# A three-stage transformer kernel: the first and the last expert in half tiles by sequence

## What is computed

```python
def reference(**kwargs):
    attn_out = _attn_ref(**attn_kwargs)      # decayed linear attention, 8 heads of 64
    x = attn_out.transpose(0, 2, 1, 3).reshape(B, S, H * D)
    x = _moe_ref(x=x, **moe_kwargs)          # 8 experts, one for each token
    return _moe2_ref(x=x, **moe2_kwargs)     # 4 softmax attentions, the best 2 mixed

# _moe_ref, for each token s of sequence b:
            e = fresh_e if (s == 0 or local_gate[b, s] < 0.5) else prev_e
            h = np.maximum(x[b, s] @ w1[e], 0.0)
            out[b, s] = p[e] * (h @ w2[e])
```

## Time and profile before

| | us |
|---|---|
| median of 3 runs | 450.05 (449.87 to 450.38) |
| the profiled execution, its time | 451.0 |
| the same, its span from first to last instruction | 449.5 |
| PE busy in it | 409.4 (91%) |
| DVE, ACT, POOL busy | 255.6, 220.8, 78.3 |

### The profile page before, as it was taken

One profiled execution on the slowest core, in us unless ns is written; L12 is line 12 of the kernel. 1 busy time (PEld: TensorE's weight loads), 2 busy tenths in 40 slices (PEclk: granted clock), 3 DMA queues, 4 the chain that ended last, 5 costly groups with the idle time before them and its releaser, 6 DMA issues.

```text
span 449.5 us, 9492 instructions
## 1 busy us (share of the span) xinstructions
PE 409.4 (91%) x3224; PEld 365.5 (81%) x3225; DVE 255.6 (57%) x493; ACT 220.8 (49%) x460; POOL 78.3 (17%) x100
## 2 busy tenths in 40 slices
PE   6998896298999999999999999299899899989987
PEld 5887784297999999898989897299887789987875
DVE  1766777776464646464646465236777531677750
ACT  3644443254464645454545455134666553466643
POOL 1011112111010100000000000540178400025330
PEclk9999997579999999999999999789999999999999
DMA  8967693777877677767766850462200021220003
GB/s 263 364 184 244 210 399 162 244 248 237 280 240 263 232 260 240 253 234 271 233 234 233 267 201 23 135 170 71 71 1 2 1 95 49 70 70 0 0 0 140
DMA packets 32392, 77.47 MB, mean 172 GB/s; under 512 B 3824, under 2 KB 4080, under 8 KB 32368
## 3 DMA queue, kind: packets, MB, share of 16 engines
q1 hardware_dynamic: 25552, 57.94, 38.1%
q0 software_dynamic: 4224, 14.68, 9.5%
q10 hardware_dynamic: 2592, 4.53, 2.7%
HBM read 56.17 MB, written 17.83 MB: 165 GB/s over the span
## 4 chain that ended last, share of the span: by engine, by line
PE 75%; issue 11%; DMA 6%; DVE 3%; POOL 2%; ACT 1%; POOLq 1%; SPq 0%; ACTq 0%; DVEq 0%
PE bank L1220 7%; PE bank L1221 6%; PE bank L1222 6%; PE bank L1207 6%; PE bank L1206 6%; PE bank L1205 6%; PE bank L1324 5%; PE bank L1309 4%; PE bank L1291 3%; PE bank L1295 3%; PE bank L1266 2%; PE bank L1265 2%; PE bank L1267 2%; POOL tokens_by_expert L446 2%; DMA tokens_by_expert<-zero 2%
## 5 line engine op out<-in xcount | busy, mean ns | idle before, releaser
L1205 PE MATMUL bank<-xh,w1h 128*128 128x256 f32 x256 | 73.6, 288 | 0.9 <-DVE xl L886 0.9
L1206 PE MATMUL bank<-xl,w1h 128*128 128x256 f32 x256 | 73.5, 287 | 0.0
L1207 PE MATMUL bank<-xh,w1l 128*128 128x256 f32 x256 | 73.5, 287 | 0.0
L880 DVE TENSOR_TENSOR w2l<-raw,w2h 128x1024 fp32r<-128x1024 f32 x32 | 37.1, 1221 | 42.6 <-ACT w2h L560 42.6
L560 ACT ACTIVATE w2h<-raw 128x1024 fp32r<-128x1024 f32 x32 | 31.7, 1051 | 47.6 <-PE bank L1222 45.7
L1205 PEld LDWEIGHTS bank<-xh,w1h 128*128 128x128 f32 x256 | 50.3, 196 | 1.3 <-DVE xl L886 1.0
L1220 PE MATMUL bank<-w2h,hh 128*128 128x512 f32 x128 | 50.7, 396 | 0.0
L1206 PEld LDWEIGHTS bank<-xl,w1h 128*128 128x128 f32 x256 | 50.2, 196 | 0.3
L1207 PEld LDWEIGHTS bank<-xh,w1l 128*128 128x128 f32 x256 | 50.2, 196 | 0.0
L1222 PE MATMUL bank<-w2h,hl 128*128 128x512 f32 x128 | 49.9, 390 | 0.0
L1221 PE MATMUL bank<-w2l,hh 128*128 128x512 f32 x128 | 49.9, 389 | 0.0
(11 more groups left out here) (159 smaller groups left out, 859.8 us busy)
## 6 DMA issues: line engine op xcount, KB each, us to landing
raw<-in_w SPq DMA_DIRECT2D x64, 512.0 KB, 6.0
tokens_by_expert<-zero POOLq DMA_DIRECT2D x8, 512.0 KB, 6.2
xr<-tokens_by_expert POOLq DMA_DIRECT2D x8, 512.0 KB, 4.0
outputs_by_expert<-ysb ACTq DMA_DIRECT2D x16, 256.0 KB
kt_in<-in_kT SPq DMA_DIRECT2D x12, 256.0 KB
q_in<-in_qT SPq DMA_DIRECT2D x12, 256.0 KB
out<-osb SPq DMA_DIRECT2D x12, 256.0 KB, 2.0
v_in<-in_vR SPq DMA_DIRECT2D x11, 256.0 KB, 5.2
```

The lines of the kernel that those rows point to most:

```text
L880: dve.tensor_tensor(part(low), raw[:, q, :], part(high).bitcast(F32), ALU.subtract).then_inc(w_lo, 1)
L1205: pe.matmul(to, w1h[:, dc, at], xh[:, dc, :], start=(dc == 0), stop=False)
L1206: pe.matmul(to, w1h[:, dc, at], xl[:, dc, :], start=False, stop=False)
L1207: last = pe.matmul(to, w1l[:, dc, at], xh[:, dc, :], start=False, stop=(dc == DC - 1))
```

## The change

- Places: expert 7's tokens of sequence 0 and of sequence 1 go to two regions; expert 0's tokens of sequence 1 begin at row 128 at the earliest, so that its first 128 rows hold tokens of sequence 0 only. There are nine units (NU = 9) instead of eight experts: expert 0, experts 1 to 6, expert 7 for sequence 0, expert 7 for sequence 1. Units 0, 7 and 8 are taken in half tiles of 128 tokens, the others in tiles of 256 as before. The routing numbers have three links more in DVE's chain and tables of 99 entries instead of 48.
- The first half tile: SP loads it when sequence 0's six scatters have landed, and then expert 0's w1 into `raw` and w2 into `first_w2` (the place of `w2l`). PE turns it before the last block's output and multiplies it by the unsplit weights in full fp32, with the tokens as the stationary operand: 8 products of 512 columns for h (`first_h`) and 8 for y (`first_y`), spread between the last products of stage A and behind them. Since h now comes out with tokens on the partitions, ACT writes relu(h) to `hs` and PE turns it (`turn_hidden`, 4 transposes for each half of the hidden columns).
- A half tile of the loops (`half_loop`) is 24 split products of 512 columns for h, 8 transposes of `hs`, 8 of the next tile, and 24 products for y. The first 4 of the hidden transposes stand after 18 of the h products, the others after 3 of the y products.
- `ys` is two tensors, one for each sequence, in the order of tokens' places without gaps. Each tile is stored to both (unit 8 to sequence 1's alone), and a tile's surplus rows are overwritten by the next tile's store, so stores wait for the one before. The five zero fills of `ys` that SP issued in stage A go to POOL, behind its first tile load (`clear_outputs`).
- ACT's `tile_out` now stands at the end of an expert's turn, behind the next w1 pieces and ahead of the next w2 pieces; it waits for both parts of y and issues two stores of 512 KB.
- POOL gathers sequence 0's rows when unit 7 is stored, sequence 1's when unit 8 is.
- Sequence 0's six blocks are turned into six banks instead of two: PE turns four of them (`AHEAD`), then the others between the values' products.

```diff
@@ -191,11 +237,15 @@
...
+        first_w2, w2l = sb_twice("first_w2", "w2l", [P, FB, D])
...
+        first_x, xh = sb_twice("first_x", "xh", [P, DC, TILE])
...
+        first_hidden, hh = sb_twice("first_hidden", "hh", [P, FB, TILE])
@@ -378,33 +445,41 @@
...
+            for j in range(C):
+                sp.wait_ge(scattered[j], 16)
+            sp.dma_start(xr[:, 0, :], rows(xs, 0, P)).then_inc(first_tile_in, 16)
             for q in range(4):
                 load_w1(0, q)
...
-                sp.wait_ge(scattered[s], 16 * NB // XRING)
-            sp.dma_start(xr[:, :, :], rows(xs, 0, TILE).rearrange("(a p) n -> p a n", p=P)).then_inc(first_tile_in, 16)
+            for q in range(4):
+                src = rows(w2, q * 2 * P, 2 * P).rearrange("(a p) n -> p a n", p=P)
+                sp.dma_start(first_w2[:, 2 * q:2 * q + 2, :], src).then_inc(first_w2_in[q], 16)
+            for j in range(C, NB):
+                sp.wait_ge(scattered[j], 16)
+            sp.wait_ge(tileT_done, 2)
+            sp.dma_start(xr[:, 0, :], rows(xs, P, P)).then_inc(second_tile_in, 16)
+            sp.wait_ge(h_done, 4)
+            for q in range(4):
+                sp.wait_ge(w_lo, q + 1)
+                load_w1(1, q)
             sp.wait_ge(pads_ready, 1)
-            r = sp.value_load(pad_i[0:1, 0:1], min_val=0, max_val=E * REGION - TILE)
@@ -447,47 +524,65 @@
...
+                    if first:
+                        with pool.If(j == 0):
+                            clear_outputs()
...
+            def clear_outputs():
+                for k in range(4):
+                    pool.dma_start(rows(ys[0], S + k * 2 * CLEAR, 2 * CLEAR).rearrange("(p a) n -> p (a n)", p=CLEAR),
+                                   zero[0:CLEAR, :]).then_inc(ys_cleared, 16)
+                pool.dma_start(rows(ys[1], B * S, P), zero[:, 0:D]).then_inc(ys_cleared, 16)
...
+            pool.wait_ge(ey_stored, 32 * tb + 32)
+            pool.sem_inc(all_stored, 1)
+            pool.wait_ge(all_stored, 1)
             gather(0)
+            pool.wait_ge(ey_stored, 32 * tb + 16 * nt + 32)
+            pool.sem_inc(all_stored, 1)
+            pool.wait_ge(all_stored, 2)
@@ -543,95 +639,164 @@
...
+            def first_hi(q):
+                act.wait_ge(raw_in[q], 16)
+                act.activation(w1h[:, q, :], raw[:, q, :], ACT.Copy).then_inc(w_hi, 1)
+
+            half_hi(0, 2, first_x)
             kept(len(GROUPS) - 2)
+            first_hi(0)
             token_rows(NB - 1)
+            first_hi(1)
             kept(len(GROUPS) - 1)
...
+            first_hi(2)
...
+            def tile_out(before, row):
+                act.wait_ge(ey_stored, 32 * before)
+                act.wait_ge(ey_done, 2 * before)
                 for th in range(TH):
...
                     act.activation(ysb[:, th, :], bank[:, 6 + th, :], ACT.Copy).then_inc(ey_ready, 1)
...
+                act.wait_ge(ey_ready, 2 * before)
+                for y in ys:
+                    act.dma_start(rows(y, row, TILE).rearrange("(a p) n -> p a n", p=P), ysb[:, :, :]).then_inc(ey_stored, 16)
...
+            hidden_rows(0, 0)
+            first_hi(3)
+            hidden_hi(0, 0, first_hidden)
+            hidden_rows(0, 1)
+            hidden_hi(0, 1, first_hidden)
+            for q in range(4):
+                at = slice(2 * q, 2 * q + 2)
+                act.wait_ge(first_w2_in[q], 16)
+                act.activation(w2h[:, at, :], first_w2[:, at, :], ACT.Copy).then_inc(w_hi, 1)
+            act.wait_ge(ey_done, 2)
+            half_hi(1, 4, xh)
+            half_out(1, 0, ys, 32)
             act.wait_ge(route_ready, 1)
-            tile_hi(0)
...
+            def half_loop(u, into):
+                tb, nt, at = loop_of(u)
...
+                with act.Fori(0, nt) as j:
+                    g = act.snap(tb + j)
...
+                    hidden_rows(g, 0)
+                    hidden_hi(mb + j, 0, hh)
+                    hidden_rows(g, 1)
+                    tile_hi(g + 1)
+                    hidden_hi(mb + j, 1, hh)
+                return lambda: half_out(act.snap(tb + nt), row_at(at + P * nt - P, P), into, act.snap(stored(nt)))
...
+            last_out = half_loop(0, ys)
+            for q in range(4):
+                hi(1, q, w1h, 0)
+            act.wait_ge(ys_cleared, 80)
+            last_out()
             act.wait_ge(prob_step, 1)
             act.activation(exps[:, :, :], exps[:, :, :], ACT.Exp).then_inc(exps_ready, 1)
...
+            with act.Fori(1, E - 1) as e:
                 for q in range(4):
                     hi(e, q, w2h, 1)
+                tb, nt, at = loop_of(e)
...
                 for q in range(4):
                     hi(e + 1, q, w1h, 0)
...
+                tile_out(act.snap(tb + nt), row_at(at + TILE * nt - TILE, TILE))
+
+            for q in range(4):
+                hi(E - 1, q, w2h, 1)
+            last_out = half_loop(NU - 2, ys)
             act.wait_ge(m2_in, 32)
             act.activation(m2h[:, :, :], m2w[:, :, :], ACT.Copy).then_inc(m2_hi, 1)
             act.activation(woh[:, :, :], wor[:, :, :], ACT.Copy).then_inc(m2_hi, 1)
...
-            tile_out(act.snap(tb + nt))
...
+            last_out()
+            last_out = half_loop(NU - 1, ys[1:])
+            last_out()
@@ -885,9 +1067,38 @@
...
                 lo(0, q, w1h, w1l, 0)
-            tile_lo(0)
+            half_lo(1, 4)
+            for q in range(4):
+                at = slice(2 * q, 2 * q + 2)
+                dve.wait_ge(w_hi, 4 + q + 1)
+                dve.wait_ge(ey_done, 2)
+                dve.tensor_tensor(w2l[:, at, :], first_w2[:, at, :], w2h[:, at, :].bitcast(F32),
+                                  ALU.subtract).then_inc(w_lo, 1)
@@ -1162,20 +1379,77 @@
...
+                if i == NB - 1:
+                    pe.wait_ge(state_ready, states_before(i))
+                    pe.wait_ge(first_tile_in, 16)
+                    turn_half(0, 2)
                 chunk_out(i)
...
+            def first_h(a, z):
+                for n in range(a, z):
+                    f, dc = n // DC, n % DC
+                    if f == 0:
+                        pe.wait_ge(raw_in[dc], 16)
+                    ins = pe.matmul(bank[:, f, :], first_x[:, dc, 0:P], raw[:, dc, f * D:(f + 1) * D],
+                                    start=(dc == 0), stop=(dc == DC - 1))
+                    if dc == DC - 1:
+                        ins.then_inc(h_done, 2)
...
+            def turn_hidden(m, f):
+                pe.wait_ge(hs_ready, 2 * m + f + 1)
+                for c in range(4):
+                    fb = 4 * f + c
+                    last = pe.transpose(bank[:, 2 + f, c * P:(c + 1) * P], hs[:, fb * P:(fb + 1) * P], ident)
+                last.then_inc(hT_done, 1)
...
+            def first_y(fbs):
...
+                    last = pe.matmul(bank[:, 6, :], first_hidden[:, fb, 0:P], first_w2[:, fb, :],
+                                     start=(fb == 0), stop=(fb == FB - 1))
...
+            pe.wait_ge(xh_ready, 2)
             turn_fresh(last_g - 1)
+            first_h(0, 1)
             rows_and_gates(NB - 1)
             turn_places(last_g - 2)
+            first_h(1, 2)
             turn_fresh(last_g)
             turn_places(last_g - 1)
+            first_h(2, 4)
             turn_places(last_g)
...
+            first_h(4, 6)
+            turn_hidden(0, 0)
+            first_h(6, 8)
@@ -1186,14 +1460,51 @@
...
-            pe.wait_ge(first_tile_in, 16)
-            turn_tile()
+            pe.wait_ge(pads_ready, 1)
+            first_y(range(0, 1))
+            turn_hidden(0, 1)
+            first_y(range(1, 6))
+            pe.wait_ge(second_tile_in, 16)
+            pe.wait_ge(xrow_ready, NB)
+            turn_half(1, 4)
+            first_y(range(6, FB))
             pe.wait_ge(route_ready, 1)
             pe.wait_ge(delta_ready, 1)
-            pe.matmul(bank[:, 7, 0:E], ones[0:1, 0:P], over[0:1, 0:E], start=True, stop=True).then_inc(ey_done, 1)
...
+            def half_loop(u, e):
...
+                    for f in range(2):
+                        for kind in range(3):
+                            for dc in range(DC):
+                                if f == 1 and kind == 1 and dc == 2:
+                                    turn_hidden(mb + j, 0)
+                                last = half_h(kind, f, dc)
+                        last.then_inc(h_done, 2)
+                    pe.wait_ge(tile_in, 16 * g)
+                    turn_tile()
+                    pe.wait_ge(ey_ready, 2 * g)
+                    half_y(e, g, range(0, 1))
+                    turn_hidden(mb + j, 1)
+                    half_y(e, g, range(1, FB))
+
+            half_loop(0, 0)
@@ -1221,14 +1532,16 @@
...
+            half_loop(NU - 2, E - 1)
+            half_loop(NU - 1, E - 1)
@@ -1244,13 +1557,13 @@
...
-            for t in range(C + 2):
-                if t < C:
-                    turn_x2(0, t)
-                if t == 2:
-                    pe.wait_ge(m2_lo, 2)
-                if t >= 2:
```

(8 more changed lines are left out.)

418 lines of the change are left out of this document (286 added, 132 removed).

## The result

Nine runs of the changed kernel took 454.02 us in the median (452.98 to 456.5), nine of the kernel before 450.05 (447.92 to 453.05). The ratio is 1.0081, with a 95% interval of 1.0055 to 1.0108: **slower by 0.8%**, where 438.7 us (433.5 to 445) had been predicted. The profiled execution took 452.98 us, its span is 451.1 us (before: 449.5).

The account below looks back on a forecast made before the run. PE was taken as the bound, busy except at the expert stage's two borders. Opening -10.4, last expert +6.7, closing -10.55 and clock +3.0 gave -11.3 from 450.05: 438.7 us, range 433.5 to 445.

Parts of the forecast that it names:

- The start of the half tile: Opening: fp32 products at 0.91 us, some in attention-stage gaps, clock at full; expert 0's split half tile starts at 92.75.
- The step that failed: Opening: after the last hidden copy (101.35), w1's split pieces (3.9 and 1.2) let expert 1 start at 106.6, 10.4 earlier.
- The tile's load: Opening: next tile's load, issued about 94, is just in time at 4 us; at 8.65 PE waits up to 4.
- a wait for `xr` at 98: Opening: listed sign that the prediction is wrong, PE waiting for the next tile's load at its turn.
- The middle experts: Six experts between the borders: PE instructions unchanged, 23.32 us each, doubled stores hidden; expert 7 starts at 246.5.
- The rival of late weights: Middle experts: ACT's new order and doubled stores delay weights, 2.6 us per expert, +15, giving 454; chance 0.05.
- The last expert: Expert 7: two half tiles of 12.6 plus `hs` waits of 2.85 and 1.9, sum 30.0; y ends at 276.5, +6.7.
- The closing: After expert 7: sequence 0's gathers run beside its second half; Q and K start 12.9 us later at 289.4, -10.55.
- I take one such loss: Last expert or closing: one fall of PE's clock, 3 us, the closing the likelier place; chance 0.40.
- The rivals: Whole kernel: no clock loss (0.27), two losses or series costs (0.22), late weights (0.05), extra half tiles (0.01).
- all that I don't see: Whole kernel: something cheaper or dearer that the prediction does not name; chance 0.05.
- the upper end: Whole kernel: 445 us, from two clock losses, fp32 products at 1.07 (+1.9) and one series cost.

Follow-up runs that it names:

- e9: Changed kernel: delta copy, zero fills and register loads (units 0, 7, 8) earlier, expert 7's first half tile reordered, hh's second half before next split; 437.17 us, ratio 0.972.
- e1: Changed kernel with one edit: DVE copies delta out of the bank before expert 0's half tile, not behind the gate chain; 436.96 us, ratio 0.985.
- e11: Changed kernel with fp32 products of zeros in PE's waits: six in that for delta, three in that for `hs` in expert 7; ratio 0.997.
- e3: Changed kernel with delta copied early and the zero fills of SP and POOL issued earlier; ratio 0.984.
- e6: Changed kernel with delta copied early, zero fills early and ACT's three register loads of expert 0 ahead of the second half tile's copy; 434.61 us, ratio 0.979.
- e10: The kernel of e9 without the zero fills moved, which stand where the changed kernel has them; ratio 0.978.
- e12: The kernel of e9 with the last half tile's five register loads at expert 1, beside those of the half tile before; 429.84 us, ratio 0.966.
- e5: The changed kernel itself run once more, without an edit; 445.42 us, ratio 1.002.

## Why the prediction was wrong

Its milestones, in us of each trace; e9 is the kernel with all edits on the same footing (stage A as long as in the first trace):

| | predicted | changed kernel | all edits (e9) |
|---|---|---|---|
| split half tile starts | 92.75 | 92.37 | 91.49 |
| wait for the next tile's load | 0 | 2.27 | 0 |
| expert 1 starts | 106.6 | 115.50 | 106.17 |
| expert 7 starts | 246.5 | 256.91 | 247.26 |
| its y ends | 276.5 | 290.76 | 275.17 |
| Q and K start | 289.4 | 305.54 | 288.46 |
| span | 438.2 (with 3 for the clock) | 451.1 | 434.0 |

- **The start of the half tile** was right: fp32 products took 0.86 us (0.91 taken), `first_h` lies in gaps of stage A, and the clock stays at full.
- **The step that failed** is "Expert 1's w1 can be split only after the last hidden copy (101.35): four ACT pieces 3.9, the last DVE piece 1.2: expert 1 starts at 106.6". It followed the data of expert 1's products and took the last low part for the last thing that PE waits for. PE's own line ahead of the loop, the wait for delta, was left out, and with it everything that DVE does behind the low parts. From the low parts' end at 110.41 to the start it is 5.1 us, and the h part then loses 1.6 to the clock. e1 shows it: with the copy moved, expert 1 starts 0.15 us behind the last low part and the h part takes 11.61; e11 shows the clock's share by itself. Under it lies a trap for readers of traces: before, DVE made the same copy behind the same links, but PE needed it only for expert 0's y part, some 10 us later (copied at 91.17), and the wait had no row at all.
- **The tile's load** ("If it takes 4 us it is just in time"): it took 4.78 but was issued at 96.06, not 94, since the fill took 6.00 us; and the wait of 2.27 cost clock as well. This was on the list of what would show the prediction wrong ("a wait for `xr` at 98"). The low parts of w1 ended 3.8 us later than 106.6. With the missed wait, that makes the 10.4 us between 246.5 and 256.91: 3.8 + 5.1 + 1.6 for the h part (13.10 for 11.52), less 0.1 in the middle experts.
- **The middle experts** were right: 23.30 apart (23.32), with twice the stores. The rival of late weights did not occur in them; expert 1 alone is longer (24.1 to 24.9) in e3, e6, e9 and e10, though not in e1 and e12.
- **The last expert** was undersized: 33.85 against 30.0. The two waits for `hs` had their sizes (4.9 together, 4.75 predicted). The rest is the lost clock (1.6) that the sum had put aside as one term, the wait of 1.00 that came back in e11, and two half tiles that take 13.0 each beside their waits (e5; 12.8 where nothing waits, in e12 from 256.00 to 268.81), not 12.6. Some 0.3 us are left over.
- **The closing** had its size where it is undisturbed: 12.9 predicted, 12.87 in e5 (280.59 to 293.46), 14.8 in the first trace, of which 1.26 is the wait at 304.03; its cause stays open. Its clock was not lost in any trace, though it holds 1.91 us of transposes, 1.45 idle and more transposes (the stretch from 292 to 296 above, at 1.00). On the rule of the Trainium skill that transposes do not count as work for the clock (TensorE: Matmul & The Clock Gate, Part 4: PE-mode transpose), this stretch should have been the likelier loss; the traces don't bear that out.
- **The clock**: "I take one such loss". There were three, with the waits of 2.27, 6.00 and 3.13 us. The first of these waits was in the sum with nothing, the second not in the text at all.
- **The rivals**: none gave the reason. The time of the slowest (454) was met by another mechanism, and 5% for all that I don't see was too little for a border with so many waits.
- **Its arithmetic** slips in two places, neither of which bears on the failure: 101.35 + 3.9 + 1.2 is 106.45, not 106.6, and the terms of the upper end (438.7, a second loss of 3, 1.9 and 2.4) make 446, not 445.

The sum of errors: 10.4 in the opening, 3.85 in the last expert, 1.9 in the closing, less the 3 for the clock, which the measured stretches already contain: 13.1 us, from -11.3 to +1.8 at the start of Q and K.
